# Attention, a four-expert mixture and an eight-expert mixture on one core: the second batch's attention is placed between the first expert's products

## What is computed

```
batch, n_heads, seq, head_dim = (2, 8, 768, 64)
for c in range(nc):                      # chunks of 32 queries
    k_full = concat(mem_k, k[c_start-16 : c_end+8])
    scores = scale * q_c @ k_full.T      # 32 queries x 64 keys
    a = exp(scores - max); a = a / (sum(a) + 1e-09)
    out[c] = a @ v_full
...
# _moe_ref: N, D, E, F = (1536, 512, 4, 1024)
for e in range(E):
    h = np.maximum(x @ w1[e], 0.0)
    out += p[:, e:e + 1] * (h @ w2[e])
# _moe2_ref: the same with 8 experts and gates P from
for _ in range(8):
    P /= P.sum(1, keepdims=True) + 1e-09
    P /= P.sum(0, keepdims=True) + 1e-09
    P *= N / E
```

## Time and profile before

| what | value |
|---|---|
| median of 3 runs | 1640.93 us (1640.2 to 1644.79) |
| time of the profiled execution | 1642.65 us |
| its span | 1640.4 us |
| PE busy | 1592.4 us, 97% of the span |
| DVE, ACT, POOL busy | 55%, 42%, 40% |
| DMA | 115.50 MB, mean 70 GB/s |
| first product begins | 91.55 us after the span's start |

### The profile page before, as it was taken

How to read it: one execution, slowest core, us unless ns; L and a number is a source line. 1 busy time by engine, 2 the same in 40 slices (tenths; PEclk the granted TensorE clock), 3 DMA queues, 4 the chain that set the end, 5 groups by cost and what they waited for, 6 DMA issues and landing times.

```text
span 1640.4 us, 21453 instructions
## 1 busy us (share of the span) xinstructions
PE 1592.4 (97%) x8692; PEld 1443.8 (88%) x8692; DVE 905.5 (55%) x1342; ACT 686.5 (42%) x1059; POOL 663.5 (40%) x536
## 2 busy tenths in 40 slices
PE   7669999999999999999999999999999999999999
PEld 6669989989899889889999989988899899899897
DVE  5645555563555564775555555557555555555553
ACT  6644344443343443434434334345343443443441
POOL 5623435432434543344343443544434434334331
PEclk9879999999999999999999999999999999999999
DMA  8512222211222221121221221221322222222221
GB/s 161 109 61 78 65 65 77 65 52 52 75 68 64 68 74 52 52 64 56 87 64 52 90 65 52 90 65 52 117 64 65 69 73 65 66 76 65 64 78 39
DMA packets 150227, 115.50 MB, mean 70 GB/s; under 512 B 22632, under 2 KB 120936, under 8 KB 150128
## 3 DMA queue, kind: packets, MB, share of 16 engines
q1 hardware_dynamic: 150128, 114.13, 23.9%
HBM read 110.96 MB, written 3.15 MB: 70 GB/s over the span
## 4 chain that ended last, share of the span: by engine, by line
PE 90%; DVE 4%; ACT 2%; issue 1%; DMA 1%; SPq 1%; POOL 1%; DVEq 0%; POOLq 0%; ACTq 0%
PE banks L504 29%; PE banks L506 29%; PE banks L505 29%; DVE s_lo L843 1%; PE banks L578 1%; DMA w_raw<-in_q 1%; DVE banks L856 1%; PE banks L490 1%; DVE t_lo L848 1%; ACT s_hi L696 1%; ACT h_hi L720 0%; DVE rows L878 0%; ACT part L716 0%; DMA v_bd<-in_v 0%; PE banks L570 0%
## 5 line engine op out<-in xcount | busy, mean ns | idle before, releaser
L422 POOL TENSOR_TENSOR w_lo<-w_raw,w_hi 128x1024 fp32r<-128x1024 f32 x96 | 315.7, 3288 | 752.0 <-ACT w_hi L701 752.0
L504 PE MATMUL banks<-t_lo,s_hi 128*128 128x384 f32 x1344 | 459.0, 342 | 20.3 <-DVE s_lo L843 10.0
L506 PE MATMUL banks<-t_hi,s_lo 128*128 128x384 f32 x1344 | 456.4, 340 | 0.0
L505 PE MATMUL banks<-t_hi,s_hi 128*128 128x384 f32 x1344 | 455.8, 339 | 0.0
L504 PE MATMUL banks<-w_lo,h_hi 128*128 128x512 f32 x1152 | 449.8, 390 | 0.0
L505 PE MATMUL banks<-w_hi,h_hi 128*128 128x512 f32 x1152 | 449.3, 390 | 0.0
L506 PE MATMUL banks<-w_hi,h_lo 128*128 128x512 f32 x1152 | 448.9, 390 | 0.0
L716 ACT ACTIVATE part<-banks 128x384 f32<-128x384 f32 x384 | 187.7, 490 | 623.8 <-PE banks L506 623.6
L856 DVE TENSOR_TENSOR banks<-banks,part 128x384 f32<-128x384 f32 x384 | 207.0, 561 | 326.8 <-ACT part L716 187.6
L720 ACT ACTIVATE h_hi<-banks 128x384 fp32r<-128x384 f32 x384 | 186.3, 492 | 261.2 <-DVE banks L856 261.2
L878 DVE SCALAR_TENSOR_TENSOR rows<-banks,gate,rows 128x512 f32<-128x512 f32 x258 | 190.2, 748 | 173.0 <-PE banks L506 172.8
(11 more groups left out here) (96 smaller groups left out, 669.4 us busy)
## 6 DMA issues: line engine op xcount, KB each, us to landing
w_raw<-in_moe_w SPq DMA_DIRECT2D x192, 256.0 KB, 3.1
w_raw<-in_moe_w SPq DMA_DIRECT2D x48, 1024.0 KB, 5.5
w_raw<-in_q SPq DMA_DIRECT2D x8, 384.0 KB, 4.6
k_in<-in_k SPq DMA_DIRECT2D x8, 384.0 KB
out_x<-rows SPq DMA_DIRECT2D x12, 256.0 KB, 3.6
v_bd<-in_v SPq DMA_DIRECT2D x16, 184.0 KB, 5.1
v_bd<-in_mem_v SPq DMA_DIRECT2D x16, 48.0 KB
v_bd<-in_v SPq DMA_DIRECT2D x32, 4.0 KB, 5.9
```

The source lines that it names most:

```text
L422: pool.tensor_tensor(out=w2_lo[m % 2][:, fs, :], in0=w2_raw[:, fs, :], in1=w2_hi[m % 2][:, fs, :].bitcast(F32), op=ALU.subtract).then_inc( ...
L504: pe.matmul(out_, lhs_hi, rhs_lo, start=start, stop=False, skip_group_check=chained)
L505: pe.matmul(out_, lhs_hi, rhs_hi, start=False, stop=False, skip_group_check=chained)
L506: return pe.matmul(out_, lhs_lo, rhs_hi, start=False, stop=stop, skip_group_check=chained)
```

## The change

The work of the kernel stays, with four edits.

1. **Place.** After unit 3, TensorE begins the first job. The steps of units 4 to 7 stand between its products and downs. `EARLY` lists 34 places: quads 0 and 1 (14 products), the six downs of m = 0, quads 2 and 3. A unit begins every 8 places.
2. **Turning.** `order_q` and `order_k` are gone. `turn_q` and `turn_k` are ordinary f32 matmuls of each head with the identity, on two 64-column tiles of the array, 16 in place of 8.
3. **Buffers.** An expert's two halves m = 0 and m = 1 use the same place of `h` and `w2` (`half_at`). Units 4 to 7 all use place 0 of `q_in`, `k_in`, `q_t`, `probs` and of `v_bd`, and unit 3's v waits for `attend(1)`, where it waited for `attend(0)`. `k_bd` gets explicit waits for the scores before.
4. **Start of a pass.** At the first quad of passes 1 to 3 DVE does `add` and `hidden` of the first block ahead of token factor 6 and of the last `accumulate` of the quad before.

The diff, cut to its core (constants, then SP's, TensorE's, ACT's and DVE's lists):

```diff
+        EARLY = [(q, i) for q in (0, 1) for i in range(PRODUCTS)] + [(-1, t) for t in range(ST)] + [
+            (q, i) for q in (2, 3) for i in range(PRODUCTS)]
+        LATER = 4
+        W2_SPLIT = {6: (0, 0), 9: (0, 1), 22: (1, 0), 26: (1, 1)}
+        UNIT_AT = {u: 8 * (u - PAIRS) for u in range(PAIRS, UNITS)}
+        TURN_Q = {max(at - 4, 0): u for u, at in UNIT_AT.items()}
+        TURN_K = {max(at - 1, 1): u for u, at in UNIT_AT.items()}
+        SCORES = {at + 3: u for u, at in UNIT_AT.items()}
+        EXPS = {at + 5: u for u, at in UNIT_AT.items()}
+        TURN_PROBS = {at + 6: u for u, at in UNIT_AT.items()}
+        ATTEND = {at + 8: u for u, at in UNIT_AT.items()}
+        TURN_X = {at + 10: u for u, at in UNIT_AT.items()}
...
+        def half_at(m):
+            return 0 if m < 2 else (m + 1) % 2
+        PLACE = [0, 1, 0, 1, 0, 0, 0, 0]
+        V_PLACE = [0, 1, 2, 1, 0, 0, 0, 0]
...
+            load_qk(2)
+            load_v(2)
+            load_w1(0)
+            load_qk(3)
+            load_v(3)
...
                 for r in range(ROWTOK):
-                    mm = pe.transpose(q_ps[u][:, r * P:r * P + QROWS], q_rows[:, r, :, :].rearrange("p h d -> p (h d)"),
-                                      ident[0:QROWS, 0:QROWS])
+                    for hh in range(2):
+                        mm = pe.matmul(q_ps[u][hh * D:hh * D + D, r * P:r * P + QROWS], q_in[PLACE[u]][:, hh, r, :],
+                                       ident[0:QROWS, 0:QROWS], start=True, stop=True, tile_position=(0, hh * D))
...
+                if u == PAIRS - 1:
+                    product(0, 0)
                 turn_x(u)
...
+            for place, (quad, i) in enumerate(EARLY):
+                beside(place)
+                if quad < 0:
+                    down(0, i)
+                elif place:
+                    product(quad, i)
...
+                if i == 2 and quad >= 0:
+                    keep_part(quad, 1)
+                    if quad > 0:
+                        split_s(quad + 1)
+                if i == 3 and quad >= 0:
+                    keep_part(quad, 2)
+                    if quad == 0:
+                        split_s(1)
...
+                if i == 4 and quad >= 0:
+                    split_s(quad + 1)
+                    add(quad, 1)
...
+                new_tokens = quad in [QUADS * f for f in FIRST[1:PASSES]]
+                if quad > LATER and not new_tokens:
                     accumulate((quad - 1) // 2 - 1, TILES_BEHIND * ((quad - 1) % 2) + 2)
                 gates(quad, 0)
                 add(quad, 0)
                 next_tokens(quad, 0)
                 hidden(quad, 0)
+                if new_tokens:
+                    split_t(pass_of(quad // QUADS), PRODUCTS - 1)
+                    accumulate((quad - 1) // 2 - 1, TILES_BEHIND * ((quad - 1) % 2) + 2)
```

More of the change, by code:

```diff
@@ L514, in product @@
                     else:
-                        pe.wait_ge(x_taken, UNITS)
+                        pe.wait_ge(kbd_even, PAIRS)
+                        pe.wait_ge(kbd_odd, PAIRS)
+                        pe.wait_ge(shifted, PAIRS)
+                if quad == 2 and i in (0, 5):
+                    pe.wait_ge(y_taken, 5 if i == 0 else 6)
                 if quad == QUADS * FIRST[p]:
@@ L597, in _, with beside @@
             turn_q(2)
-            for u in range(UNITS):
+            for u in range(PAIRS):
                 turn_probs(u)
-                if u + 2 < UNITS:
+                if u + 2 < PAIRS:
                     turn_k(u + 2)
                 attend(u)
-                if u + 2 < UNITS:
+                if u + 2 < PAIRS:
                     scores(u + 2)
-                if u + 3 < UNITS:
+                if u + 3 < PAIRS:
                     turn_q(u + 3)
+                if u == PAIRS - 1:
+                    product(0, 0)
                 turn_x(u)
-            for quad in range(ALLQ):
+            def beside(place):
+                if place in TURN_Q:
+                    turn_q(TURN_Q[place])
+                if place in TURN_K:
+                    turn_k(TURN_K[place])
+                if place in SCORES:
+                    scores(SCORES[place])
+                if place in TURN_PROBS:
+                    turn_probs(TURN_PROBS[place])
+                if place in ATTEND:
+                    attend(ATTEND[place])
+                if place in TURN_X:
+                    turn_x(TURN_X[place])
+            for place, (quad, i) in enumerate(EARLY):
[4 more added lines that the diff above has]
+                    product(quad, i)
+            beside(len(EARLY))
+            for quad in range(LATER, ALLQ):
                 m = quad // 2 - 1
@@ L768, in _, with beside @@
-            for quad in range(ALLQ):
+            def beside(place):
+                if place in TURN_Q:
+                    copy_q(TURN_Q[place])
+                if place in TURN_K:
+                    copy_k(TURN_K[place])
+                if place in EXPS:
+                    exps(EXPS[place])
+                if place in TURN_PROBS:
+                    copy_probs(TURN_PROBS[place])
+                if place in TURN_X:
+                    take_x(TURN_X[place])
+            split_t(0, 1)
@@ new lines, in _ @@
+            for place, (quad, i) in enumerate(EARLY):
+                beside(place)
+                if place < 4:
+                    split_t(0, (2, 6, 4, 5)[place])
+                if i == 0 and quad > 0:
+                    keep_part(quad, 0)
+                if i == 1 and quad >= 0:
+                    hidden(quad, 0)
+                if i == 2 and quad >= 0:
[7 more added lines that the diff above has]
+                if i == 4 and quad >= 0:
+                    keep_part(quad, 3)
+                if i == 5 and quad >= 0:
+                    hidden(quad, 1)
+                if i == 6:
+                    hidden(quad, 2)
+                    hidden(quad, 3)
+                if place in W2_SPLIT:
+                    split_w2(*W2_SPLIT[place])
```

383 lines of the change are left out of this document (222 added, 161 removed).

## The result

| what | before | after |
|---|---|---|
| median | 1640.57 us (1638.48 to 1644.79, 4 runs) | 1615.11 us (1613.22 to 1616.35, 4 runs) |
| ratio after / before | | 0.9846, interval 0.9825 to 0.9868 |
| profiled execution, its span | 1642.65, 1640.4 us | 1616.35, 1614.6 us |
| product (0, 0) begins | 91.55 us | 48.35 us (forecast 46.3) |
| quad 4 begins | 152.75 us | 140.72 us (forecast 131.4) |

The changed kernel is 25.5 us faster; the forecast was 31. Its median lies inside the forecast's own 1603 to 1616 us, at the upper end. Over the study the kernel before had medians of 1640.6, 1641.05 and 1642.8 in three groups of runs, the changed one 1615.1 and 1616.3 in two.

What follows compares the result with a forecast made beforehand. Bound: TensorE with all its matmuls in a row, plus a front of 91.55 us in which it can't begin them. Quad 4 earlier 21.4 + boundaries 10 = 31.4 us off 1642.65: 1611.3, median about 1610; range 1599 to 1625.

Steps and rivals of the forecast that it cites:

- The turning: `turn_q` and `turn_k` as matmuls on two 64-column tiles side by side: 1.65 us each for q and k.
- the two bounds: For a turning on two overlapping tiles: 1.5 us if columns bound it, 1.65 us if weight loads do.
- Rival one: The two 64-column tiles do not overlap: 3.0 us a turning, 16 us more in all, 1626 us; chance 12%.
- Product (0, 0): First product on TensorE begins near 46.3 us, where it began at 91.55.
- Just in time, and the first thing to be late: v of unit 3, waiting for `attend(1)`, is shared by 44.6 us, ahead of `attend(3)` at 44.7.
- The stream to quad 4: From product (0, 0): products 29.2, downs 16.4, `turn_x(3)` 0.7, four units 30.8, waits 8; quad 4 at 131.4 us.
- The drain: Array drain at a change of tiling mode: no large one seen; at 0.2 us a step 5 us, left to the range.
- The waits for `s_lo`: Ahead of quads 1 and 2: neither 4.92 us wait is left, none over 1 us.
- The boundaries: Three pass boundaries: `add` 2.5 us earlier at each, 7.5, plus some 2.5 from cold stretches behind the first two: 10 us.
- The rival of a fallen clock: Small steps and short waits keep TensorE at 1.2 GHz from 46 to 131 us: 39 us lost, 1649; chance 3%.
- The front: All ahead of quad 4: it begins at 131.4 us in place of 152.75, 21.4 us earlier.
- The rival of in-order queues (1621): Late unit steps on ACT and DVE pass on: waits twice 8 us, v of unit 3 late by 3: 11 us; 20%.

Runs made afterwards that it cites:

- the second execution: The changed kernel run once more, unedited: 1616.32 us against 1642.84 for the kernel before, ratio 0.984.
- the second probe: Changed kernel with extra unread matmuls behind products of some quads: 16 on 64-column tiles, 24 on 32-column tiles, both in a row: 1.667, 1.636, 3.108 us a product.

## Why the prediction was right, and where its sizes were off

- **The turning: right.** Two 64-column tiles work side by side: one after the other would take 3.0 us. A step takes 1.47 us from start to start in the stream and 1.667 with its way in and out (measured between products); forecast 1.65. The choice between the two bounds was made for the wrong reason: the price is that of the columns and of the visit. A matmul of 128 columns takes 0.219 on a tile, so 8 of 96 columns on each of two tiles 8 x 0.75 x 0.219 = 1.31 us, and 0.35 is left for the visit. Rival one is out.
- **Product (0, 0): right within some 2 us.** 48.35 and 45.91 us in two executions, forecast 46.3; 45.9 to 50.1 over six with this order of loads. Of the 2.4 us between the two, 1.55 is the stretch at 1.2 GHz behind the wait for q of unit 3, and 0.9 a later start of `turn_q(3)`. The prediction had q land near 29 as well, and priced neither the slow stretch nor the spread of the load. "Just in time, and the first thing to be late" was wrong: `share_v` of unit 3 ended at 45.35, 1.5 us ahead of `attend`.
- **The stream to quad 4: the term that was too small.** Forecast 85.1 us, measured 92.4 in both executions (92.37 and 92.44). Of the 7.3 us, 1.4 to 1.6 are waits (9.4 and 9.6 for 8). The single waits came much as named: 0.75 behind `scale_x(3)` (forecast 0.5), 1.09 for `copy_q` (0.9), 0.74 for the k copy (1.0), 2.18 for a token factor (1.8), 0.80 for `copy_probs(4)` (1.2), 1.26 for `exps(5)` (1.6), and 2.5 for the rest (1), most of it one wait of 1.99 for the last unit's `exps`. The other 5.7 (82.8 for 77.1), read in the second execution: the steps of each of the four units come to 7.95 us with their ways in and out (2 x 1.667, `scores` 1.636, `attend` 1.66, two full-array steps of 0.66) for 7.7, so 1.0 us in all; the eight waits hide 0.07 to 0.18 us each, since a row counts idle time from the modelled end, where the next start would have come that much earlier, 1.2; two stretches at 1.2 GHz (starts of product matmuls 0.32 apart, a `scores` of 1.78 and an `attend` of 1.84 in place of 1.45), an estimated 2.7; some 0.8 is not assigned. The kernel of the second probe has the same list up to quad 4, and its execution had no slow stretch there (product (0, 0) to quad 4, clock 1.00):

```profile
48.95:139.21 90.26, 80.41 (x939) 68.49 (x935) 59.99 (x94) 45.63 (x68) 43.02 (x31) 1.00 0.39 97
```

Beside 9.8 us of waits that leaves 80.5 us, 2.3 less than 82.8. So the two slow stretches cost some 2.3 to 2.7 us, and 0.8 to 1.2 is not assigned; 0.2 of it may be `turn_k`, priced here like `turn_q` though it has 100 columns for 96 (1.52 for 1.47 in the rows). None of these terms was large. The sum had none for the hidden part of a wait and for the slow stretches, and kept the visits outside.

- **The drain: seen, and mostly paid already.** The prediction let it stand outside the sum at 0.2 us a step, 5 us. It is 0.33 us a visit to small tiles, more than that; but the price of `scores`, 1.52, holds 24 / 4 x 0.219 = 1.31 us of columns, so 0.21 of it was in; the 1.65 of the turning, taken for another reason, held it whole. That reading, "changes in and out included, so no large drain is seen", was wrong about its size and nearly right about its cost.
- **The waits for `s_lo`: right.** 0.2 us is left of 9.8.
- **The boundaries: right.** Forecast 10, measured 10.8 in the profiles and 10.2 by the run without edit 4. The remaining wait is 0.83, forecast 0.4: the prediction split 3.92 us evenly on two token factors, 1.96 each, but the one that stays ahead of `add` takes 2.50 and the moved one 1.27, so the wait shrank by 2.1 us and not by 2.5. The stretches went from 21.46, 20.26 and 18.74 to 16.5 to 16.6 each. Some 2.1 us of each is the wait, and the first two give back a slow stretch, as was said; it was 4.2 us in this execution of the kernel before, forecast 2.5, and 1.4 and 3.1 in two others without the edit. That the sum came out at 10.8 is in part this execution's luck.
- **Clock: right.** 0.96 and 0.97 in the stream. The rival of a fallen clock came true in two short stretches, 2.3 to 2.7 us. With the turning alone the clock of the front rose to 1.00, but the long waits for `q_rows` went at the same time, so whether matmuls in place of transposes helped it is not shown.
- **The sum.** 12.0 + 10.8 from the change, 3 from stretches whose order the change leaves alone, makes the 25.8 us between the two spans. The front was forecast at 21.4, so in these two executions the forecast was helped by 3 us that it had no reason to expect; 2.1 of them are the spread of quads 33 to 63. Medians average over such luck and give 25.5 to 26.5 us: 15.7 for front and turning, 10.2 for the boundaries. The traces put quad 4 8 to 14 us earlier, so 15.7 is more than they show ahead of it.
- **The rival of in-order queues (1621) was half true.** Its waits did not double, but the moved copy of unit 4 (`share_v`) shows its mechanism: lateness taken away at one product turned up at the next. The other half, v of unit 3 late by 3 us, did not happen.

What stays open: the 0.8 to 1.2 us that the stream's sum lacks; by how much place alone gained, since it was run only with buffers and turning (9.8 us over the turning by medians, 3.5 to 7.0 at quad 4 in the traces); and why quads 65 to 94 are 0.5 us faster.

## What to carry to other kernels

Steps of a front in which TensorE often stands idle can go between the products of the next phase, but the gain is less than the earlier start: here product (0, 0) came 43 us earlier and quad 4 12. Price a small step between large ones by its whole visit (here 1.64 to 1.67 us where the next start comes 1.45 to 1.47 behind its own), and add what the row of a wait hides, here up to 0.18 us each. When a wait is removed by moving one instruction on a strict list, look for the same wait at the next reader before counting it as gained, and don't judge 2 us by one profile; traces of other edits that leave the same stretch alone can be put together for it. At a change of phase, ask of each engine's list what the next phase's first result needs: here one split and one `accumulate` moved behind one `add` were worth some 10 us.
